# Weaving the up projection of chunk j+2 with the down projection of chunk j, matmul by matmul, in a fused attention and two-layer feed-forward kernel

## The reference

```python
def reference(**kwargs):
    attn_out = _attn_ref(**attn_kwargs)            # (4, 8, 576, 64): pooled attention + a band of 7 keys
    x = attn_out.transpose(0, 2, 1, 3).reshape(B * S, H * D)     # 2304 tokens x 512
    x = _moe_ref(x=x, **moe_kwargs)
    return _moe2_ref(x=x, **moe2_kwargs)

def _moe_ref(x, w_in, w_out):                      # w_in 512 x 2048, w_out 2048 x 512
    h = x @ w_in
    g = np.where(h > 0.0, h, np.exp(np.minimum(h, 0.0)) - 1.0)
    return g @ w_out

def _moe2_ref(x, w_in, w_out, s, b):
    r = np.maximum(x @ w_in, 0.0)
    return (s * (r * r) + b) @ w_out
```

## Time and profile before

| | us |
|---|---|
| median of 3 runs | 968.87 (968.4 to 969.43) |
| profiled execution, span from first to last instruction | 969.6 |
| PE busy in it | 910.8 (94%) |
| DVE, ACT, POOL busy | 405.1, 416.7, 150.1 |

### The profile page before, as it was taken

How to read it: one execution, slowest core, us unless ns; L and a number is a source line. 1 busy time by engine, 2 the same in 40 slices (tenths; PEclk the granted TensorE clock), 3 DMA queues, 4 the chain that set the end, 5 groups by cost and what they waited for, 6 DMA issues and landing times.

```text
span 969.6 us, 16132 instructions
## 1 busy us (share of the span) xinstructions
PE 910.8 (94%) x5936; PEld 859.2 (89%) x5936; DVE 405.1 (42%) x780; ACT 416.7 (43%) x1106; POOL 150.1 (15%) x141
## 2 busy tenths in 40 slices
PE   5676677999999999999999999999999999999998
PEld 4565666999999999999999999999999999999996
DVE  7676675432323323323224244344344343343432
ACT  7667576754434434344346632232232222232222
POOL 4444453750000000000016630000000000000000
PEclk8788798999999999999999999999999999999999
DMA  5546553430000000000014400000000000000000
GB/s 129 148 122 155 135 139 101 141 100 1 1 1 1 0 0 0 0 0 1 1 44 130 124 31 1 1 33 1 1 32 0 33 0 0 32 1 1 33 1 33
DMA packets 71185, 41.42 MB, mean 43 GB/s; under 512 B 41696, under 2 KB 62688, under 8 KB 71136
## 3 DMA queue, kind: packets, MB, share of 16 engines
q1 hardware_dynamic: 71136, 40.78, 15.1%
HBM read 36.05 MB, written 4.72 MB: 42 GB/s over the span
## 4 chain that ended last, share of the span: by engine, by line
PE 84%; SPq 11%; issue 2%; DMA 2%; DVE 1%; ACT 0%; ACTq 0%; DVEq 0%
PE ps_h L503 41%; PE ps_y L524 21%; PE ps_y L522 21%; SPq L256 3%; SPq L240 3%; SPq L250 2%; SPq L251 1%; DMA kpad<-in_kt 1%; DMA wstage<-in_w_in 1%; SPq L242 1%; PE ps_s L411 0%; SPq L252 0%; SPq L255 0%; PE ps_x L455 0%; SPq L262 0%
## 5 line engine op out<-in xcount | busy, mean ns | idle before, releaser
L644 ACT ACTIVATE g_hi<-tmp 128x384 fp32r<-128x384 f32 x192 | 101.0, 526 | 261.9 <-PE ps_y L524 152.2
L503 PE MATMUL ps_h<-xs_hi,win_late_lo 128*128 128x384 f32 x576 | 193.8, 336 | 0.0
L503 PE MATMUL ps_h<-xs_hi,win_late_hi 128*128 128x384 f32 x576 | 193.8, 336 | 0.0
L503 PE MATMUL ps_h<-xs_lo,win_late_hi 128*128 128x384 f32 x576 | 193.6, 336 | 0.0
L793 DVE TENSOR_TENSOR g_lo<-tmp,g_hi 128x384 fp32r<-128x384 f32 x192 | 107.4, 559 | 204.7 <-ACT g_hi L644 204.7
L638 ACT ACTIVATE tmp<-ps_h 128x384 f32<-128x384 f32 x192 | 94.3, 491 | 227.7 <-PE ps_h L503 225.3
L785 DVE SCALAR_TENSOR_TENSOR tmp<-tmp,ps_h 128x384 f32<-128x384 f32 x96 | 53.2, 554 | 161.8 <-ACT tmp L641 161.0
L503 PEld LDWEIGHTS ps_h<-xs_lo,win_late_hi 128*128 128x128 f32 x576 | 108.3, 188 | 3.3
L503 PEld LDWEIGHTS ps_h<-xs_hi,win_late_hi 128*128 128x128 f32 x576 | 108.2, 188 | 3.2
L503 PEld LDWEIGHTS ps_h<-xs_hi,win_late_lo 128*128 128x128 f32 x576 | 108.3, 188 | 0.0
L789 DVE TENSOR_TENSOR tmp<-tmp 128x384 f32<-128x384 f32 x96 | 55.2, 575 | 121.9 <-ACT tmp L638 121.9
(11 more groups left out here) (94 smaller groups left out, 1469.2 us busy)
## 6 DMA issues: line engine op xcount, KB each, us to landing
wstage<-in_w_in SPq DMA_DIRECT2D x32, 256.0 KB, 2.8
wstage<-in_w_out SPq DMA_DIRECT2D x32, 256.0 KB, 2.8
qbd<-in_qt SPq DMA_DIRECT2D x32, 144.0 KB, 3.6
kpad<-in_kt SPq DMA_DIRECT2D x16, 288.0 KB, 3.8
v<-in_v SPq DMA_DIRECT2D x16, 288.0 KB
out<-wstage SPq DMA_DIRECT2D x18, 256.0 KB, 2.2
vwin<-in_v SPq DMA_DIRECT2D x32, 112.0 KB
vwin<-in_v SPq DMA_DIRECT2D x32, 33.5 KB
```

What stands on the lines that cost most here:

```text
L503: mm = pe.matmul(o, w_chunk(0, a, j)[:, c * P:(c + 1) * P], xs[x][:, slot, c, :], start=(c == 0 and p == 0), stop=(c == CH - 1 and p == 2))
L644: act.activation(g[0][:, j % 2, :], x, ACT.Copy).then_inc(hi_ready, 1)
```

## The change

Only PE's order changes. The bodies of `up` and `down` are cut into single passes, and a new function `both` issues one pass of up(j+2) and then its share of down(j): one down pass behind each up pass in layer 0, nine over twelve up passes in layer 1. Chunk 0 of each block keeps the old form, up(2) whole and then down(0) whole. In the last block down(14) and down(15) stay alone. The waits are the same ones; that on `g_ready` now stands behind the first up pass.

```diff
+            def both(layer, n, j, un, uj, slot):
+
+                downs = 3 * (CH if layer == 0 else NO)
+                up_start(layer, un, uj)
+                for k in range(3 * CH):
+                    up_pass(layer, un, uj, slot, k)
+                    if k == 0:
+                        down_start(layer, n, j)
+                    for d in range(k * downs // (3 * CH), (k + 1) * downs // (3 * CH)):
+                        down_pass(layer, n, j, d)
 
             def blocks(layer, n, slot, next_slot, last):
                 for j in range(J):
-                    if j + 2 < J:
+                    if j == 0:
                         up(layer, n, j + 2, slot)
+                        down(layer, n, j)
+                    elif j + 2 < J:
+                        both(layer, n, j, n, j + 2, slot)
                     elif not last:
-                        up(layer, n + 1, j + 2 - J, next_slot)
-                    down(layer, n, j)
+                        both(layer, n, j, n + 1, j + 2 - J, next_slot)
+                    else:
+                        down(layer, n, j)
```

More of the change, by code:

```diff
@@ L491, in _, with up_start @@
             pairs(pe, step)
-            def up(layer, n, j, slot):
+            PASSES = ((0, 0), (0, 1), (1, 0))
+            def up_start(layer, n, j):
                 t = STEPS * layer + J * n + j
@@ L497, in up, with up_pass, down_start @@
                 pe.wait_ge(act_ready, t + 1)
[L498 to L507, removed]
+            def up_pass(layer, n, j, slot, k):
+                c, p = k // 3, k % 3
+                a, x = PASSES[p]
+                if j == 0 and p == 0:
+                    pe.wait_ge(x_split, CH * (NB * layer + n) + c + 1)
+                mm = pe.matmul(ps_h[:, j % 4, 0:TB], w_chunk(0, a, j)[:, c * P:(c + 1) * P], xs[x][:, slot, c, :],
+                               start=(k == 0), stop=(k == 3 * CH - 1))
+                if k == 3 * CH - 1:
+                    mm.then_inc(up_ready, 1)
+            def down_start(layer, n, j):
                 t = STEPS * layer + J * n + j
@@ L510, in down @@
                 pe.wait_ge(g_ready, G_CREDIT + t + 1)
[L511 to L524, removed]
@@ L525, in down, with down_pass @@
-                mm.then_inc(g_used, 1)
+            def down_pass(layer, n, j, k):
+                last = 3 * (CH if layer == 0 else NO) - 1
+                c, p = k // 3, k % 3
+                a, x = PASSES[p]
+                if j == 0 and p == 0:
+                    if c < 2:
+                        pe.wait_ge(act_evac, 2 * (NB * layer + n) + c + 1)
+                    elif layer == 0:
+                        pe.wait_ge(dve_evac, 2 * n + c - 1)
+                    else:
+                        pe.wait_ge(dve_evac, E_CREDIT + 2 * NB + n)
+                go = dict(start=(j == 0 and p == 0), stop=(j == J - 1 and p == 2))
+                if layer == 0:
+                    mm = pe.matmul(ps_y[:, c, 0:TB], w_chunk(1, a, j)[:, c * P:(c + 1) * P], g[x][:, j % 2, :], **go)
+                else:
+                    mm = pe.matmul(ps_y[:, c, 0:DM], g[a][:, j % 2, c * P:(c + 1) * P], w_chunk(1, x, j), **go)
+                if k == last:
+                    mm.then_inc(g_used, 1)
@@ new lines, in up, with down @@
+            def up(layer, n, j, slot):
+                up_start(layer, n, j)
+                for k in range(3 * CH):
+                    up_pass(layer, n, j, slot, k)
+            def down(layer, n, j):
+                down_start(layer, n, j)
+                for k in range(3 * (CH if layer == 0 else NO)):
+                    down_pass(layer, n, j, k)
+            def both(layer, n, j, un, uj, slot):
+                downs = 3 * (CH if layer == 0 else NO)
+                up_start(layer, un, uj)
+                for k in range(3 * CH):
+                    up_pass(layer, un, uj, slot, k)
+                    if k == 0:
+                        down_start(layer, n, j)
+                    for d in range(k * downs // (3 * CH), (k + 1) * downs // (3 * CH)):
+                        down_pass(layer, n, j, d)
```

## The result

The changed kernel takes 978.67 us (median of 4 runs, 978.04 to 979.79) against 969.15 us before (4 runs, 968.40 to 969.78). The ratio is 1.0105, 95% interval 1.0093 to 1.0118: 1% slower, 9.5 us.

What follows compares the result with a forecast made beforehand. PE was taken as the bound, with no waits in the layers. Stalls of 7.4 us at block changes and 1.7 us at layer ends sum to 9.1 us, on 968.87 us giving 978.0 us, range 972 to 990 us.

Steps and rivals of the forecast that it cites:

- The bound: Both layers: PE busy in every microsecond from 180 to 965 us, so the change can't remove a wait.
- The passes priced at nothing: 3960 passes that change neighbours: weaving itself costs nothing, since turns from up to down show the usual spacing.
- Inside a block: Woven steps between block changes: activation needs 3.14 us of 4.7 us, 1.5 us are left, so nothing is lost.
- the sign: In the changed kernel's timeline, twelve woven passes of each kind should take 4.16 us; another time makes the forecast wrong.
- Where a block changes: down(0) waits for the first ps_y copy: 0.66 us in layer 0, once 1.18, 0.71 in layer 1; 7.4 us in sum.
- The handover: From the release of PE to regular passes again: 0.05 + 0.12 = 0.17 us at each stall.
- the change to block 5: Last block change of layer 0: a weight write of 0.52 us before the copies makes the stall 1.18 us.
- The layer ends: down(15) waits for g_lo at the end of each layer: 0.86 + 0.81 = 1.7 us.
- The sum: Whole kernel: 7.4 + 1.7 = 9.1 us more, 978.0 us as median, 978.7 us as span of the profiled execution.
- More spacing in this order: Rival: woven passes all take 0.18 us, 28 us more, 1006 us in all; chance 0.06.
- The clock: Rival: twelve gaps of about 0.7 us pull the granted clock lower, 42 us more, 1020 us in all; chance 0.04.
- Faster through another PSUM tile at each pass: Rival: writing one tile twice in a row keeps passes slow; weaving gains at most 56 us, 922 us; chance 0.05.

Runs made afterwards that it cites:

- copies_first_tail_whole: The changed kernel with the copies out of ps_y moved ahead of chunk 1's activation and the last pair of each layer unwoven; 969.94 us, ratio 1.0004.
- all_but_last_pair: The changed kernel with all pairs woven but the 12 ahead of a block change or layer end; 969.99 us, ratio 1.0006 to before.
- weave_by_3: The changed kernel woven in threes, three up passes and then the downs that belong to them; 977.48 us, ratio 1.0105 to before.
- chunk0_woven: The changed kernel with chunk 0 of every block woven too, up(2) with down(0); 1008.91 us, ratio 1.0427 to before.
- copies_first: The changed kernel with the copies out of ps_y moved ahead of chunk 1's activation on ACT and DVE; 972.25 us, ratio 1.0029 to before.

## Why the prediction was right

**The bound.** PE was the only bound and had no waits to lose, so the change could not gain by removing one. The profile after bears it out: a pair of projections takes no less time in it than before, 4.16 us in layer 0 and 4.18 in layer 1.

**The passes priced at nothing.** Nearly right. In the layers, weaving alone added 0.45 us (copies_first_tail_whole) or 0.52 us (all_but_last_pair), 0.0001 us per pass. The turns from up to down in the trace before were a fair sample for this order. That they need not be one for every order is what weave_by_3 showed. There I took the price for nothing again, and missed by 4 us.

**Inside a block** nothing was lost, as forecast: between two changes there is no hole, and the same 60 us, from 236 to 296, hold 348 passes after and 347 before. The prediction gave 4.16 us for a pair in both layers, and called itself wrong if a pair took another time. In layer 1 it was 4.18. But there it had been 4.17 before (2.08 + 2.09 by its own numbers), so this was a slip in writing down the sign and not a cost of the weaving.

**Where a block changes.** 0.66 us was forecast and 0.65 measured in layer 0 (once 0.71), 0.71 forecast and 0.68 or 0.74 measured in layer 1. The handover, called the softest term and taken from one case, came out as assumed: 0.05 us from the end of the copy to PE (302.05 to 302.10), and 0.11 us more until the next pass (0.28 for 0.17). At the change to block 5, with the weight write in between, 1.18 was forecast. The timeline of PE in the kernel after:

```profile
503.55 0.34 PE L506 MATMUL ps_h<-xs_hi,win_early_lo 128*128 128x384 f32 x1
504.87 0.41 PE L530 MATMUL ps_y<-g_hi,wout_early_hi 128*128 128x384 f32 x1 [0.99 <-ACT xy L686]
505.12 0.33 PE L530 MATMUL ps_y<-g_lo,wout_early_hi 128*128 128x384 f32 x1
```

1.57 less 0.35 is 1.22 us. The ten together were forecast at 7.4 us, and their sum by the starts is 7.4; taking them away gave back 7.5.

**The layer ends** were forecast at 0.81 us for layer 1. Measured in the kernel after:

```profile
968.71 0.39 PE L532 MATMUL ps_y<-wout_late_hi,g_lo 128*128 128x512 f32 x1
969.71 0.48 PE L532 MATMUL ps_y<-wout_late_hi,g_hi 128*128 128x512 f32 x1 [0.60 <-DVE g_lo L827]
970.02 0.39 PE L532 MATMUL ps_y<-wout_late_lo,g_hi 128*128 128x512 f32 x1
```

1.31 less 2 x 0.232 is 0.85 us. Layer 0 had 0.96 against 0.86. Both ends came to 1.8 against 1.7.

**The sum**, 9.1 us, stands against 9.5 us in the medians and 9.75 in the layers. What it lacks is the spacing, about 0.5 us, and a tenth of a us at the ends. The span of the profiled execution, forecast at 978.7, was 976.7 us: its attention was shorter by 2.7 us (first pass at 160.61 instead of 163.30), so a sum against a span holds only for the part that the change touches.

**The rivals.** More spacing in this order: 0.5 us instead of 28. The clock: it did not move behind gaps of 0.65 to 1.2 us. With gaps of 2.4 to 3.2 us, in chunk0_woven, it did behind six of ten, at some 10 us in all. The prediction held the trace before, at 1.00 over eight tiles, against this rival; that showed nothing, since PE has no gap in the layers there. The section "A second HAM failure mode: psum-queue depth-cycling" of the Trainium skill's page "TensorE: Matmul & The Clock Gate" has short idles between groups swing the clock; the runs here agree for six of the ten gaps of 2.4 to 3.2 us and do not for any of 0.6 to 1.2. Faster through another PSUM tile at each pass: the spacing stayed at 0.173 us, so using one tile twice in a row is not what keeps it above 0.160. The formula that the prediction took here from the same page of the Trainium skill, section "Back-to-back issue gap", is given there for a matmul by itself, and not for a stream in which every pass has its weight load, so its 162.5 ns was no measure for this kernel.

No version here beats the kernel before. The best woven ones are even with it, since they only give back what the weaving lost.

## What to carry to other kernels

Weaving two phases on the engine that is the bound makes both end together. The consumer of the phase that used to end first then gets its data later by nearly a phase, while the engine's next use of that consumer's result can be due as before. So before weaving, write down for each handover when the producer ends, how long the chain behind it takes, and when the result is due, at the seams (block changes, ends) above all, for the steady state can have 1.5 us to spare where a seam comes out 0.7 us short. If one seam is short, leave the pair ahead of it whole, which gave the whole loss back here (all_but_last_pair). Or move the consumer's urgent work ahead of what can wait, which gave back the 7.5 us of the block changes (copies_first); the layer ends, where there was nothing to move, still needed their pair whole.

## What the runs showed of the hardware

At the lower clock level the passes of 384 columns stood 0.32 us apart (306.67, 306.99, 307.31 in chunk0_woven), which is 384 cycles at 1.2 GHz, and those of 512 columns in layer 1 0.43 us, which is 512 cycles. At the upper level they stood at 0.173 and 0.232, where 384 and 512 cycles at 2.4 GHz are 0.160 and 0.213. So the 8% or 9% that a float32r pass takes beyond its columns shows only at the upper level. It would fit something that is fed or drained at a rate which does not double with the clock, but that is a guess that no run here tests.

A gap of 2.4 to 3.2 us in dense work brought a stretch of 3.4 us at the lower level behind six times of ten, gaps up to 1.2 us never, in this kernel and the variants above.
